# Narrow warm-up matmuls, tiles between scores and output, earlier row decays and later differences in a fused retention and mixture kernel

## The reference

```python
def _attn_ref(q, k, v):                       # B, H, S, D = 2, 8, 576, 64
    scores = 1.0 / np.sqrt(D_) * np.matmul(q, k.transpose(0, 1, 3, 2))
    gamma = 1.0 - 2.0 ** (-5.0 - np.arange(H))
    rel = pos[:, None] - pos[None, :]
    Dmat = np.where(rel >= 0, gamma[:, None, None] ** rel[None, :, :], 0.0)
    return np.matmul(scores * Dmat[None], v)

def _moe_ref(x, domain_probs, w1, w2):        # x: 1152 x 512, 4 experts, F = 1024
    p = domain_probs / (domain_probs.sum(-1, keepdims=True) + 1e-09)
    for e in range(E):
        out += p[:, e:e + 1] * (np.maximum(x @ w1[e], 0.0) @ w2[e])
    return out

def _moe2_ref(x, w_in, w_out):                # F = 2048
    h = x @ w_in
    return (h * np.tanh(np.log1p(np.exp(h)))) @ w_out
```

## Time and profile before

| | us |
|---|---|
| median of 3 runs | 621.67 |
| lowest and highest | 620.61, 621.79 |
| the profiled execution | 622.52 |
| its span, first to last instruction | 620.7 |
| PE busy | 605.9 (98%) |
| POOL busy | 278.2 (45%) |
| DVE busy | 264.0 (43%) |
| ACT busy | 234.7 (38%) |

### The profile page before, as it was taken

One profiled execution on the slowest core, in us unless ns is written; L12 is line 12 of the kernel. 1 busy time (PEld: TensorE's weight loads), 2 busy tenths in 40 slices (PEclk: granted clock), 3 DMA queues, 4 the chain that ended last, 5 costly groups with the idle time before them and its releaser, 6 DMA issues.

```text
span 620.7 us, 9829 instructions
## 1 busy us (share of the span) xinstructions
PE 605.9 (98%) x4016; PEld 547.0 (88%) x4016; DVE 264.0 (43%) x361; ACT 234.7 (38%) x434; POOL 278.2 (45%) x230
## 2 busy tenths in 40 slices
PE   6799999999999999999999999999999999999997
PEld 4699799999999999999999999989989999989996
DVE  2467654423154434154534154535545432324334
ACT  2464433322323332223432123435455454334431
POOL 2658645535335544435552535532446553443300
PEclk9699999999999999999999999999999999999999
DMA  8963202332112331112322112321211232201002
GB/s 345 331 213 109 80 35 68 104 101 68 35 35 68 103 103 57 46 35 68 102 84 62 58 34 69 102 69 37 67 34 49 69 105 84 68 1 52 1 1 101
DMA packets 24923, 50.47 MB, mean 81 GB/s; under 512 B 2864, under 2 KB 2992, under 8 KB 24880
## 3 DMA queue, kind: packets, MB, share of 16 engines
q1 hardware_dynamic: 24736, 49.84, 25.1%
q10 hardware_dynamic: 144, 0.02, 0.0%
HBM read 47.49 MB, written 2.36 MB: 80 GB/s over the span
## 4 chain that ended last, share of the span: by engine, by line
PE 92%; DVE 2%; ACT 2%; issue 1%; DMA 1%; POOL 1%; SPq 0%
PE bank L494 30%; PE bank L496 29%; PE bank L495 29%; PE bank L442 1%; DMA loaded<-in_feats 1%; PE bank L470 1%; PE bank L612 1%; PE bank L474 1%; ACT xt L736 0%; ACT w_hi L368 0%; DVE acc_sb L888 0%; DVE acc_sb L892 0%; POOL w_lo L395 0%; DVE xs_a L962 0%; DVE xs_a L959 0%
## 5 line engine op out<-in xcount | busy, mean ns | idle before, releaser
L395 POOL TENSOR_TENSOR w_lo<-w_raw,w_hi 128x512 fp32r<-128x512 f32 x96 | 134.6, 1416 | 149.8 <-ACT w_hi L368 149.8
L494 PE MATMUL bank<-w_hi,h_hi 128*128 128x512 f32 x432 | 168.7, 391 | 0.0
L496 PE MATMUL bank<-w_hi,h_lo 128*128 128x512 f32 x432 | 168.3, 390 | 0.0
L495 PE MATMUL bank<-w_lo,h_hi 128*128 128x512 f32 x432 | 168.3, 390 | 0.0
L875 DVE TENSOR_TENSOR h_act<-part,bank 128x384 f32<-128x384 f32 x96 | 52.9, 551 | 169.9 <-PE bank L496 169.4
L390 POOL TENSOR_TENSOR ws<-ws_f,ws 128x1024 fp32r<-128x1024 f32 x24 | 57.6, 2401 | 145.1 <-ACT ws L364 145.1
L496 PEld LDWEIGHTS bank<-w_hi,h_lo 128*128 128x128 f32 x432 | 81.1, 188 | 16.9
L495 PEld LDWEIGHTS bank<-w_lo,h_hi 128*128 128x128 f32 x432 | 81.1, 188 | 12.3
L494 PEld LDWEIGHTS bank<-w_hi,h_hi 128*128 128x128 f32 x432 | 81.0, 188 | 12.1
L722 ACT ACTIVATE part<-bank 128x384 f32<-128x384 f32 x72 | 35.3, 491 | 138.6 <-PE bank L496 138.6
L842 DVE SCALAR_TENSOR_TENSOR h_lo<-h_act,h_hi 128x384 fp32r<-128x384 f32 x64 | 73.2, 1153 | 20.5 <-ACT h_hi L712 19.9
(11 more groups left out here) (88 smaller groups left out, 863.0 us busy)
## 6 DMA issues: line engine op xcount, KB each, us to landing
w_raw<-in_weights SPq DMA_DIRECT2D x144, 256.0 KB, 2.7
loaded<-in_toks SPq DMA_DIRECT2D x9, 512.0 KB, 7.0
loaded<-in_feats SPq DMA_DIRECT2D x8, 512.0 KB, 6.2
out<-acc_sb SPq DMA_DIRECT2D x6, 256.0 KB, 2.1
out<-acc_sb SPq DMA_DIRECT2D x1, 768.0 KB, 3.5
loaded<-in_first SPq DMA_DIRECT2D x1, 726.0 KB, 4.4
ident<-in_ident SPq DMA_DIRECT2D x1, 64.0 KB, 5.0
p_nat<-in_probs ACTq DMA_DIRECT2D x1, 18.0 KB, 5.1
```

The source lines that it names most:

```text
L395: pool.tensor_tensor(w_lo[layer][:, x], w_raw[:, r % RAW], w_hi[layer][:, x].bitcast(F32), ALU.subtract).then_inc(s_wl, 1)
L494: pe.matmul(out, w[0], x[0], start=first, stop=False, **more)
L495: pe.matmul(out, w[0], x[1], start=False, stop=False, **more)
L496: return pe.matmul(out, w[1], x[0], start=False, stop=last, **more)
```

## The change

- The warm-up is 72 matmuls of 64x64 zeros ahead of the first scores, and none behind them. It was 7 and 5 matmuls of 128x512.
- Tiles 0, 1, 2, 4 and 5 stand between `scores_and_state(c)` and `output(c)` (`TILE_AMID`), tiles 3, 6 and 7 behind `output(c)` (`TILE_AFTER`). All stood behind it.
- Four of the weight jobs of the turns stand one turn later (`JOBS_IN`).
- The row decays are made in turns 0 to 3; they were made in turn 0 and in turns 4 to 7.
- At the end of the part, DVE makes the differences of x ahead of tile 7's low part and of the last `first_lo`, with the first `t_lo` among them. ACT does the two weight jobs of stage 1 ahead of the four `t_hi`, and `t_hi` waits for the differences in their new order.

```diff
-TILES_IN = {3: (0,), 4: (1,), 5: (2, 3), 6: (4,), 7: (5, 6), 8: (7,)}
-JOBS_IN = {1: (("w1", 0, 0),), 2: (("w1", 0, 1), ("w1", 0, 2)), 3: (("w1", 0, 3),), 4: (("w1", 0, 4), ("w1", 0, 5)),
...
+TILE_AMID = {3: 0, 4: 1, 5: 2, 6: 4, 7: 5}
+TILE_AFTER = {5: 3, 7: 6, 8: 7}
+JOBS_IN = {2: (("w1", 0, 0), ("w1", 0, 1)), 3: (("w1", 0, 2),), 4: (("w1", 0, 3), ("w1", 0, 4)),
...
-ROWS_IN = {4: 5, 5: 6, 6: 7, 7: 8}
+ROWS_IN = {0: (2, 3), 1: (4, 5), 2: (6,), 3: (7, 8)}
-WARM_START, WARM_NEXT = 7, 5
+WARM = 72
...
-                    pe.matmul(banks[7][:, :], zeros[:, 0:P], zeros[:, :], start=True, stop=True)
+                    pe.matmul(banks[7][HALF[0], 0:CH], zeros[:, 0:CH], zeros[:, 0:CH], start=True, stop=True)
...
-            keep_warm(WARM_NEXT)
             for c in range(PLACES):
                 if has_state(c):
                     scores_and_state(c)
+                if c in TILE_AMID:
+                    early_tile(TILE_AMID[c])
                 output(c)
-                for t in TILES_IN.get(c, ()):
-                    s, i = divmod(t, ITEMS)
-                    plain_ready(s, i)
-                    plain_products(s, i, range(KT))
+                if c in TILE_AFTER:
+                    early_tile(TILE_AFTER[c])
...
-                act.wait_ge(s_tf, (9, 8, 6, 10)[n] if e else (3, 2, 1, 4)[n])
+                act.wait_ge(s_tf, (9, 8, 6, 10)[n] if e else (2, 3, 1, 4)[n])
...
+            for job in IN_STAGE[1]:
+                job_hi(act, job)
             for n in range(4):
                 t_hi(0, n)
-            for job in IN_STAGE[1]:
-                job_hi(act, job)
...
-            first_lo(PLACES - 1)
...
+            dve.wait_ge(s_xt, PLACES)
             dve.tensor_tensor(full[0], b12, b11, ALU.subtract).then_inc(s_tf, 1)
-            dve.tensor_tensor(full[2], b22, b12, ALU.subtract).then_inc(s_tf, 1)
             dve.wait_ge(s_tf, 1)
             dve.tensor_tensor(full[1], b22, full[0], ALU.subtract).then_inc(s_tf, 1)
-            dve.wait_ge(s_tf, 3)
+            plain_lo(*divmod(TILE_AFTER[PLACES - 1], ITEMS))
+            dve.tensor_tensor(full[2], b22, b12, ALU.subtract).then_inc(s_tf, 1)
+            t_lo(0, 0)
+            first_lo(PLACES - 1)
+            dve.wait_ge(s_tf, 2)
             dve.tensor_tensor(full[3], full[1], b21, ALU.subtract).then_inc(s_tf, 1)
-            dve.wait_ge(s_tf, 4)
-            for n in range(4):
+            for n in range(1, 4):
                 t_lo(0, n)
```

More of the change, by code:

```diff
@@ L53 @@
 STATE_BANK, OUT_BANK = 2, 3
-TILES_IN = {3: (0,), 4: (1,), 5: (2, 3), 6: (4,), 7: (5, 6), 8: (7,)}
-JOBS_IN = {1: (("w1", 0, 0),), 2: (("w1", 0, 1), ("w1", 0, 2)), 3: (("w1", 0, 3),), 4: (("w1", 0, 4), ("w1", 0, 5)),
-           5: (("w1", 0, 6),), 6: (("w1", 0, 7), ("w2", 0, 0)), 7: (("w2", 0, 1), ("w2", 0, 2), ("s", 0, 0)),
-           8: (("w2", 0, 3), ("w2", 0, 4)), 9: (("w2", 0, 5),)}
+TILE_AMID = {3: 0, 4: 1, 5: 2, 6: 4, 7: 5}
+TILE_AFTER = {5: 3, 7: 6, 8: 7}
+JOBS_IN = {2: (("w1", 0, 0), ("w1", 0, 1)), 3: (("w1", 0, 2),), 4: (("w1", 0, 3), ("w1", 0, 4)),
+           5: (("w1", 0, 5), ("w1", 0, 6)), 6: (("w1", 0, 7), ("w2", 0, 0)),
+           7: (("w2", 0, 1), ("w2", 0, 2), ("s", 0, 0)), 8: (("w2", 0, 3), ("w2", 0, 4)), 9: (("w2", 0, 5),)}
 WEIGHTS_IN = (2, 2, 2, 2, 2)
-ROWS_IN = {4: 5, 5: 6, 6: 7, 7: 8}
+ROWS_IN = {0: (2, 3), 1: (4, 5), 2: (6,), 3: (7, 8)}
 PROBS_IN = 5
-WARM_START, WARM_NEXT = 7, 5
+WARM = 72
 STAGES = 6
@@ L522, in plain_products, with early_tile @@
                     mm.then_inc(s_l1, 1)
+            def early_tile(t):
+                s, i = divmod(t, ITEMS)
+                plain_ready(s, i)
+                plain_products(s, i, range(KT))
             def product(s, j):
@@ L618, in keep_warm @@
                 for _ in range(count):
-                    pe.matmul(banks[7][:, :], zeros[:, 0:P], zeros[:, :], start=True, stop=True)
+                    pe.matmul(banks[7][HALF[0], 0:CH], zeros[:, 0:CH], zeros[:, 0:CH], start=True, stop=True)
             pe.wait_ge(s_zt, 1)
-            keep_warm(WARM_START)
+            keep_warm(WARM)
             pe.wait_ge(s_feats[0], landed(0))
@@ L740, in _ @@
                     first_hi(c - 1)
-                for t in TILES_IN.get(c - 1, ()):
-                    plain_hi(*divmod(t, ITEMS))
+                if c - 1 in TILE_AFTER:
+                    plain_hi(*divmod(TILE_AFTER[c - 1], ITEMS))
                 if has_state(c):
@@ L753, in _ @@
                         job_hi(act, job)
+                if c in TILE_AMID:
+                    plain_hi(*divmod(TILE_AMID[c], ITEMS))
+            for job in IN_STAGE[1]:
+                job_hi(act, job)
             for n in range(4):
                 t_hi(0, n)
-            for job in IN_STAGE[1]:
-                job_hi(act, job)
             for s in range(2, ALL_STAGES):
@@ L937, in _ @@
                     masked(c)
-                if c == 0:
-                    for i in range(2, 5):
-                        rows(i)
                 if c > 0:
@@ L946, in _ @@
                     first_lo(c - 1)
-                for t in TILES_IN.get(c - 1, ()):
-                    plain_lo(*divmod(t, ITEMS))
-                if c in ROWS_IN:
-                    rows(ROWS_IN[c])
+                for i in ROWS_IN.get(c, ()):
+                    rows(i)
+                if c - 1 in TILE_AFTER and c < PLACES:
+                    plain_lo(*divmod(TILE_AFTER[c - 1], ITEMS))
                 if c == PROBS_IN + 1:
                     probs()
-            first_lo(PLACES - 1)
+                if c in TILE_AMID:
+                    plain_lo(*divmod(TILE_AMID[c], ITEMS))
             b11, b21 = xf[:, 0:KH, 0:TC], xf[:, KH:, 0:TC]
```

## The result

The changed kernel took 626.38 us, the median of 4 runs (624.34 to 627.27), beside 621.68 us of the kernel before: a ratio of 1.0072, with a 95% interval of 1.0057 to 1.0086. The forecast was 619.4 us, with a range of 616.5 to 622.5. The change is slower by 4.7 us, and the sign of the forecast was wrong. The profiled execution took 626.3 us, its span is 624.5. In the profile before the span was 620.7, so the two profiles differ by 3.8 us. The rest of the 4.7 is the profile before, which is 0.84 us above the median of its kernel.

A forecast was written before the change was run, and what follows sets the result against it. Late fetches of 256-instruction blocks and the half clock were taken to bound the first 31 us, with TensorE busy afterwards. Gains of 1.6 (front) and 0.65 (stage end) sum to 2.25: 621.67 - 2.25 = 619.4 us, range 616.5 to 622.5.

The forecast's parts named there:

- The count of instructions: At the front, TensorE's stops come every 256 instructions and move 21, 19 and 18 matmuls into `scores_and_state(1)`, (2), (3).
- the bound of 7.9 us: Warm-up's slow case: weight loads not hidden under the short matmuls, an end at 9.2, up to 1.8 us lost.
- The rival by which the stops stay: Front: the sum of the stops is as before, only the end of stage 1 gains 0.65: 621.0 us; chance 0.23.
- The sum at the front: Late instruction blocks and work up to `scores_and_state(4)`: it begins at 29.5 instead of 31.06 us, gain 1.6 us.
- The gain stays: After `scores_and_state(4)` begins, TensorE is busy without a gap in both kernels, so the front's 1.6 us is kept.
- Tiles between scores and output: 0: Attention part: moving tiles between scores and output costs or gains 0, as TensorE waited for nothing from 31 us.
- The end of the stage: End of the first stage: TensorE's 1.12 us wait for the `part` copy goes, `h_act` is late next; gain 0.65 us.
- The step 55.4 + 11.9 + 1.9 + 1.1 = 70.3: DVE at the first stage's end: start, eight large operations, two more slow ones, two low parts; `h_act` at 70.3, not 70.92.
- the bound of -0.5 us: Worst case for the first stage's end: all eight large DVE operations slow and P1 1 us late.
- Rival 3: Front: third block later than about 25 us, half clock over tile 0 and `output(3)`, perhaps the next tile: 623.9 us; chance 0.14.
- Rival 1: Front: blocks come at 4.76 us or sooner, or full clock; gain 3.5 to 5.5, 616.0 to 617.5 us; chance 0.15.
- faster: The outcome that the changed kernel takes less time, holding the forecast and Rival 1: chance 0.62.

The follow-up runs named there:

- e13_filler: The changed kernel with seven wide matmuls of zeros right ahead of P7, in TensorE's wait: 624.14 us, ratio 1.0036.
- e2_count: The kernel before, three of seven wide warm-up matmuls replaced by 63 of one column, 60 more instructions' worth of matmuls with hardly more work: 627.34 us, ratio 1.0080.
- e11_before_again: The kernel before, unchanged, run a single time more for a second profile: 620.78 us.
- e1_warm: The kernel before with only the change's warm-up, 72 narrow matmuls ahead and none behind the first scores: 627.73 us, ratio 1.0081.
- e4_amid: The kernel before with only tiles 0, 1, 2, 4 and 5 moved between scores and output: 625.04 us, ratio 1.0053.
- e6_timed: The changed kernel with ACT's two weight jobs back behind the four `t_hi`, DVE's new order kept: 622.47 us over ten runs, ratio 1.0008.

## Why the prediction was wrong

The forecast had a gain of 1.6 us at the front, nothing in the middle, 0.65 at the end and nothing for the clock. The profiles have losses of 0.35, 1.64, 0.24 and 1.55 us.

**The count of instructions: right.** The stops came 20 and 18 matmuls into `scores_and_state(2)` and `(3)`, where 19 and 18 had been worked out, and left `of_state`. The first one, 21 into `scores_and_state(1)`, was hidden by the features in the kernel after, and stands there in `e13_filler`, 2.46 us long. `e2_count` shows the cause. The warm-up of 4.0 us took 4.05, and the bound of 7.9 us fell away. The rival by which the stops stay is refuted.

**The sum at the front: the step that failed.** It said that the third block is there at 23.8 and `scores_and_state(4)` at 29.5; measured 24.77 and 31.41. The second block, put at 17.8, came at 19.05. In the sum's own terms: the features of place 1 landed 1.2 us later, so that the block was entered at about 12.0, where 11.5 had been assumed, and the latency from there was about 7.0 us, not 6.28. Together they put the second block 1.25 us late. The third took 5.7 us more, 0.3 less than assumed. The work behind it took 6.64 us, not 5.7: the rest of the scores 1.49 (forecast 1.0) and the tile at the half clock 4.13 (3.7). That makes the 1.9 us between 29.5 and 31.41. The step that failed is to take a latency as a property of a block that can be carried over. It holds a wait until the packet begins, 4.7 us for the second block (12.0 to 16.69) and 3.3 for the third (19.05 to 22.34), and this wait changes from block to block and from one execution to the next. The 0.35 us lost lie just outside the bounds (a gain of 5.5 and a loss of 0.1), and the value taken between them had no row that it was near to. The gain of 1.6 us was also set against one profile of before; `e11_before_again` began place 4 at 28.37, so a start at 29.5 would not have been a gain for certain.

**"The gain stays" behind 31 us: failed.** The boundaries were counted to the fourth and no further. The sixth stands in `output(5)` and cost 0.76 us. The same carried on for the warm-up alone would have shown that the fifth comes behind a block with hardly any of a tile in it, the 3.35 us of `e1_warm`. "Tiles between scores and output: 0" measured 0.66 us for the two parted pairs. That place 2's low part is wanted sooner was not seen at all; `e4_amid` waited 2.35 us for it, and the change only escaped by the stop ahead of it.

**The end of the stage: right in kind, wrong in size and sign.** The 1.12 us went, and P7 waits for `part`, as forecast. The step 55.4 + 11.9 + 1.9 + 1.1 = 70.3 failed. Less the 1.99 us by which the first `second` is later, DVE starts the differences at 54.9 and `h_act` at 71.16, 0.24 later than before and not 0.6 sooner; P7 follows it by 1.53 us in both profiles. The eight large operations took 13.0 us, no more than the 13.8 forecast. What was missing are DVE's waits, put at nothing and measured 1.3 us (1.04 for tile 7's high part, which ACT makes, 0.26 for a high part of `xt`), and `first_lo(8)` with tile 7's low part took 1.9 us and not 1.1. The low part of tile 7 waited for ACT in the kernel before as well, until 57.99:

```profile
57.99 0.56 DVE L842 SCALAR_TENSOR_TENSOR h_lo<-bank,h_hi 128x384 fp32r<-128x384 f32 x1 [2.57 <-ACT h_hi L703]
```

The larger miss is ACT's part of the change. The two jobs were moved to free the copy for P6, and the five splits in a row that they set off on GpSimd were counted, but not weighed against leaving them where they were: with them back, the same order of DVE brings P7 15.08 us behind the first `second`, where before it was 16.48 (`e6_timed`), a gain of 1.4. The loss of 0.24 up to P7 is inside the bound of -0.5 us; what is outside it is the clock.

**The clock: the mechanism was a rival's, in another place.** Rival 3 had the clock slip at 25 us, by a late third block. The half clock there was about as long as before; it fell behind P7's wait instead and took 1.55 us. It is 41% of the difference between the profiles, and no term of the forecast. That it comes with the wait is likely and not shown (`e13_filler`).

**Two slips of arithmetic.** Rival 1 with its gain of 5.5 us and the 0.65 of the end comes to 615.5 us, not 616.0, and "faster" adds to 0.63. Neither moves the forecast.

## What to carry to other kernels

Count instructions as well as work. Here 256 of them lasted 2 to 4 us at the front, and the next block was there 4 to 7 us after the entry. Adding or removing some dozens at the start then moves every later stop. So carry the boundaries on to where the data queues are quiet, and check each block for a long piece of work that covers the fetch. When an operation is moved ahead on an engine with time to spare, ask which engine it sets off and what that one slows; here two operations on ACT cost 3.9 us in the median, 3.2 of it seen in the profiles through GpSimd, DVE and TensorE's clock. Take two profiles of the kernel before, before the place of a stretch is used as a term.

## What the runs showed of the hardware that was not expected

- A matmul of one column has its price in its instruction: 60 more of them cost 5.1 us in the median, by stops that stand tens of us behind them.
- A block's packet can begin long after the block before was entered. In the kernel after the block for the stop at 19.05 was transferred only at 16.7 us, although the block before it had been entered by about 12 us. The DMA share in between was 1.03. This is its line in the table of DMA queues for 16.65 to 16.75 us (packets, MB, share):

```profile
q8 instruction: 1, 0.02, 68.4%
```

- From the end of a block's packet to TensorE going on it was 1.1 to 1.6 us at every stop of every profile (1.26 for that one, 17.79 to 19.05).
- DVE's difference of 128x768 took 0.95 us alone and 2.05 us beside GpSimd's splits, which took 1.81 to 1.87 us each beside it and 1.28 alone.
- A single wait of 1.81 us amid dense work was followed by 3.3 us at half the clock in both profiles of the kernel after, though waits of 1.66 and 1.82 us in two other programs were not.
- A pair of tiles that is parted, which brings two more changes between 64x64 and 128x128 matmuls, took 0.33 us more in both places, with no idle time shown.
